# Attention sums scaled by reciprocals that a DMA spreads over the partitions, and turned once instead of twice

## The reference, cut to what matters

```python
scores = scale * (q @ k^T) + bias;  kept: keys of a local window, and a few global keys
scores = scores - max(scores)
a = exp(scores)
a = a / (sum(a, axis=-1) + 1e-9)          # one divisor per query and head
x = (a @ v), heads side by side            # (2, 768, 512)
h = (x^T @ U @ V)^T;  u = x + h            # mixes tokens, rank 32
y = u + relu(u @ w_ch1) @ w_ch2            # 512 -> 2048 -> 512
out = gated unit of y with w_in, w_spatial, b_spatial, w_out
```

## Time and profile before

| what | us |
|---|---|
| median of three runs | 494.83 |
| span of the profiled execution | 493.2 |
| profiled execution beside the median: what lies around the span | 1.6 |
| DVE takes the first sums (step 1), start | 13.84 |
| ACT copies turned exponentials of quad 2 (step 1), start | 15.56 |
| ACT copies turned exponentials of quad 22 (step 22), start | 88.37 |
| first matmul after attention, start | 92.15 |

### The profile page before, as it was taken

One profiled execution on the slowest core, in us unless ns is written; L12 is line 12 of the kernel. 1 busy time (PEld: TensorE's weight loads), 2 busy tenths in 40 slices (PEclk: granted clock), 3 DMA queues, 4 the chain that ended last, 5 costly groups with the idle time before them and its releaser, 6 DMA issues.

```text
span 493.2 us, 7961 instructions
## 1 busy us (share of the span) xinstructions
PE 489.0 (99%) x2804; PEld 409.3 (83%) x2804; DVE 310.2 (63%) x727; ACT 222.0 (45%) x520; POOL 250.2 (51%) x221
## 2 busy tenths in 40 slices
PE   9999999999999999999999999999999999999997
PEld 8788677887888888888888888888888888998986
DVE  5888788421279456564655656557868888878600
ACT  7988889532234633242332322415433356333122
POOL 5997576443346666854566546232885201950000
PEclk9999999999999999999999999999999999999999
DMA  8734501132222322012222020220213000001022
GB/s 236 236 127 111 191 2 45 46 128 86 81 87 89 129 85 71 31 72 85 85 86 78 8 85 3 84 64 2 64 65 115 4 0 1 1 1 43 23 85 108
DMA packets 14697, 36.29 MB, mean 74 GB/s; under 512 B 2496, under 2 KB 2752, under 8 KB 14656
## 3 DMA queue, kind: packets, MB, share of 16 engines
q1 hardware_dynamic: 12640, 32.35, 19.8%
q10 hardware_dynamic: 2016, 3.41, 1.8%
HBM read 32.61 MB, written 3.15 MB: 72 GB/s over the span
## 4 chain that ended last, share of the span: by engine, by line
PE 82%; DVE 6%; POOL 4%; ACT 3%; issue 2%; DVEq 2%; DMA 1%; SPq 0%; ACTq 0%
PE bank L1792 15%; PE bank L1724 9%; PE bank L1644 9%; PE bank L1874 8%; PE bank L1821 8%; PE bank L1814 8%; PE bank L1513 7%; PE bank L1551 4%; PE bank L1569 4%; PE bank L1536 4%; PE bank L1503 1%; POOL sp_op L587 1%; PE bank L1583 1%; DVE newton L1020 1%; DVEq L1008 1%
## 5 line engine op out<-in xcount | busy, mean ns | idle before, releaser
L532 POOL TENSOR_TENSOR w_slot<-stage,w_slot 128x1024 fp32r<-128x1024 f32 x30 | 73.0, 2445 | 65.4 <-ACT w_slot L1249 65.4
L940 DVE TENSOR_TENSOR uT<-bank,uT 128x512 f32<-128x512 f32 x68 | 45.8, 689 | 25.2 <-PE bank L1821 23.2
L1179 ACT ACTIVATE prob<-prob,row_min 128x256 f32<-128x256 f32 (+1 forms) x96 | 45.9, 480 | 6.9 <-DVE row_min L756 6.8
L1792 PE MATMUL bank<-u_op,s_slot 128*128 128x512 f32 x192 | 47.6, 389 | 0.0
L1724 PE MATMUL bank<-hid,w_slot 128*128 128x512 f32 x192 | 46.9, 393 | 0.0
L1644 PE MATMUL bank<-u_split,w_slot 128*128 128x512 f32 x192 | 46.5, 391 | 0.0
L1814 PE MATMUL bank<-hid,w_slot 128*128 128x512 f32 x192 | 46.1, 389 | 0.0
L1821 PE MATMUL bank<-hid,w_slot 128*128 128x512 f32 x192 | 46.1, 389 | 0.0
L978 DVE TENSOR_TENSOR part<-part,bank 128x512 f32<-128x512 f32 x40 | 27.4, 686 | 26.9 <-PE bank L1792 26.5
L1724 PEld LDWEIGHTS bank<-hid,w_slot 128*128 128x128 f32 x192 | 35.7, 188 | 8.2 <-issue 0.9
L1814 PEld LDWEIGHTS bank<-hid,w_slot 128*128 128x128 f32 x192 | 36.0, 188 | 7.5
(11 more groups left out here) (152 smaller groups left out, 963.5 us busy)
## 6 DMA issues: line engine op xcount, KB each, us to landing
stage<-in_w_ch SPq DMA_DIRECT2D x32, 512.0 KB, 3.3
qk_raw<-in_qk SPq DMA_DIRECT2D x23, 256.0 KB, 4.7
v_all<-in_v SPq DMA_DIRECT2D x12, 256.0 KB, 5.2
out_dram<-o_stage ACTq DMA_DIRECT2D x11, 256.0 KB, 2.0
stage<-in_w_spT SPq DMA_DIRECT2D x6, 384.0 KB, 3.1
stage<-in_w_in SPq DMA_DIRECT2D x4, 512.0 KB, 4.2
stage<-in_w_out SPq DMA_DIRECT2D x2, 512.0 KB, 4.0
V_raw<-in_V SPq DMA_DIRECT2D x4, 96.0 KB, 4.6
```

The costliest lines, as they stand in the source:

```text
L532: nc.gpsimd.tensor_tensor(dst[:, LO, :], stage[n % 2][:, 0:w], dst[:, HI, :].bitcast(F32), ALU.subtract).then_inc(w_lo, 1)
L940: vec.tensor_tensor(y, y_bank(e)[:], y, ALU.add).then_inc(y_sum, 1)
L1179: last = sc.activation(prob[r][:, e, 0:w], prob[r][:, e, 0:w], ACT.Exp, bias=row_min[:, k:k + 1], scale=-1.0, accum_out=row_sum[:, q:q + 1])
L1792: last = mm(seven_bank[held][:], lhs, u_op[op][:, m, k, :], start=not more and k == 0 and p == 0, stop=k == 1 and p == 2, skip_group_check ...
```

## The change

The reciprocals of a quad are now made one step earlier, written by a DMA to a scratch tensor in DRAM, and read back by two DMAs that repeat them over 64 partitions each (`inv_rows`, 128 x 256, three buffers). DVE multiplies the bank of sums by them and writes `uT`, dims by tokens, straight away (`scale_x`). PE turns `uT` once to tokens by dims, into the same bank, and ACT copies that to `x_all` (`take_x`). The bank alternates between `o_bank` and `aux`. The first turn and the copy `oT` are gone. The mixing of the first batch moves by one step and to other banks.

```diff
+            def store_inverse(g):
+                sp.wait_ge(inv_ok, g + 1)
+                sp.dma_start(inv_dram[g, :, :].rearrange("k q -> q k"), row_inv[:, g % 4 * 4:g % 4 * 4 + 4],
+                             allow_slow_non_contiguous=True).then_inc(inv_out[g % 2], 16)
+            def spread_inverse(g):
+                sp.wait_ge(inv_out[g % 2], 16 * (g // 2 + 1))
+                if g >= 3:
+                    sp.wait_ge(xT_sb, g - 2)
+                for e in range(2):
+                    rows = slice(e * D, (e + 1) * D)
+                    sp.dma_start(inv_rows[g % 3][rows, :, :],
+                                 inv_dram[g, 2 * e:2 * e + 2, :].partition_broadcast(D)
+                                 ).then_inc(inv_in[g % 3], 16)
...
-                for t in range(3, TILES):
-                    load_qk(t)
-                    load_v(t - 1)
-                    if t == 6:
+                load_qk(3)
+                load_v(2)
+                load_v(3)
+                for g in range(QUADS):
+                    if g == 11:
+                        load_v(NT)
+                    store_inverse(g)
+                    spread_inverse(g)
+                    if g % 2 == 0 and g // 2 + 4 < TILES:
+                        load_qk(g // 2 + 4)
+                    if g in (1, 3):
+                        load_v((g + 7) // 2)
+                    if g % 2 and g >= 11 and (g + 3) // 2 < TILES:
+                        load_v((g + 3) // 2)
+                    if g == 6:
                         load_stage(0)
                         load_stage(1)
...
-            def take_oT(g):
...
-            def take_x(g):
...
+            def scale_x(g):
+                dve.wait_ge(inv_in[g % 3], 32 * (g // 3 + 1))
                 dve.wait_ge(pv_done, g + 1)
+                vec.tensor_tensor(x_tile(g), x_bank(g)[:, 0:256].rearrange("p (c q) -> p c q", c=2),
+                                  inv_rows[g % 3][:], ALU.mult).then_inc(xT_sb, 1)
...
-                    if s >= 1 and s - 1 not in OT_AMID:
-                        take_oT(s - 1)
                     if 0 <= s < QUADS and s != 2:
                         take_probT(s)
                     if s >= 1:
-                        take_x(s - 1)
-                    if 0 <= s < QUADS:
-                        invert(s)
+                        scale_x(s - 1)
+                    if 0 <= s + 1 < QUADS:
+                        invert(s + 1)
...
-            def take_xT(g, after=0):
+            def take_x(g):
                 t, hq = divmod(g, 2)
-                act.wait_ge(xT_ps, g + 1)
-                if after:
-                    act.wait_ge(x_half, after)
+                act.wait_ge(x_ps, g + 1)
+                if t == XS and hq == 0:
+                    act.wait_ge(z_acc, 1)
+                sc.activation(x_all[:, t % XS, hq * 256:hq * 256 + 256], x_bank(g)[:, 0:256],
+                              ACT.Copy).then_inc(x_half, 1)
...
                     if s == 13:
                         split_stage(0)
+                    if s == GATHER:
                         copy_z(0)
+                    if s >= 2:
+                        take_x(s - 2)
                     if 0 <= s + 1 < QUADS:
                         add_eps(s + 1)
...
-                    if s >= 2:
-                        take_xT(s - 2, s)
...
-                    if s in (16, 18, 20, 22):
-                        round_u((s - 16) // 2)
+                    for j in range(FIRST):
+                        if s == MIX_AT[j] + 1:
+                            round_u(j)
...
             def weigh(g):
-                if g:
-                    pe.wait_ge(oT_sb, g)
+                if g >= 2:
+                    pe.wait_ge(x_half, g - 1)
...
-            def turn_o(g):
...
+            def turn_x(g):
+                t, hq = divmod(g, 2)
+                pe.wait_ge(xT_sb, g + 1)
+                for c in range(2):
+                    last = nc.tensor.transpose(x_bank(g)[:, c * P:(c + 1) * P],
+                                               uT[:, 2 * hq + c, t * P:(t + 1) * P], ident[:])
+                last.then_inc(x_ps, 1)
...
```

More of the change, by code:

```diff
@@ L23, with build @@
 MASK_FILL = 1.0e9
-def build(nc, qk, qT, kT, v, cfg, U, V, w_ch, w_in, w_spT, b_sp, w_out, x_dram, out):
+def build(nc, qk, qT, kT, v, cfg, U, V, w_ch, w_in, w_spT, b_sp, w_out, x_dram, inv_dram, out):
     B, DM, S = qT.shape
@@ L161, in build @@
         z_part = at("z_part", [P, DM], F32, SLOT * 11)
-        oT = [at(f"oT{r}", [P, 2, P], F32, SLOT * 11 + 2048 + 1024 * r) for r in range(2)]
+        inv_rows = [at(f"inv_rows{r}", [P, 2, P], F32, SLOT * 11 + 2048 + 1024 * r) for r in range(3)]
         pos_w = SLOT * 11 + 2048
@@ L237, in build, with x_bank, x_tile @@
         FIRST = KD
-        z_bank, fold_bank = (s_bank[0], aux), (s_bank[2], aux)
+        z_bank, fold_bank = (s_bank[2], aux), (s_bank[0], aux)
+        def x_bank(g):
+            return (o_bank, aux)[g % 2]
+        def x_tile(g):
+            t, hq = divmod(g, 2)
+            return uT[:, 2 * hq:2 * hq + 2, t * P:(t + 1) * P]
+        GATHER = 14
+        MIX_AT = (16, 18, 20, 20)
         def mix_bank(j):
             if j < FIRST:
-                return s_bank[0]
+                return s_bank[3 if j == FIRST - 1 else 2]
             return o_bank if j >= 2 * KD and j % 2 else aux
-        OT_AMID = (0, 1, 12)
         def globs_before(g):
@@ L672, in _ @@
                         split_early(1, g // 22)
-                    if g >= 17 and g % 2:
-                        split_u((g - 17) // 2)
+                    for j in range(FIRST):
+                        if g == MIX_AT[j] + 2:
+                            split_u(j)
             with pool.Else():
@@ L885, in _ @@
                         score_bias(s + 2)
-                    if s == 14:
+                    if s == 15:
                         split_z(0)
-                    if s in (15, 17, 19):
-                        sum_u((s - 15) // 2)
-                    if s == 22:
-                        sum_u(FIRST - 1)
+                    for j in range(FIRST):
+                        if s == MIX_AT[j]:
+                            sum_u(j)
             with dve.Else():
@@ L1299, in _ @@
                     round_u(j)
-                for g in range(2 * NT, QUADS - 2):
-                    take_xT(g)
+                for g in range(2 * NT, QUADS):
+                    wide_take_xT(g)
+                act.wait_ge(w_xT, QUADS)
+                act.sem_inc(xT_sb, QUADS)
+                act.sem_inc(x_half, QUADS - 2)
             for f in range(FT):
@@ L1686, in _ @@
                 hidden(0)
-                turn_o(QUADS - 1)
-                pe.wait_ge(x_half, QUADS - 1)
                 turn_x(QUADS - 2)
@@ L1697, in _ @@
                 for g in range(2 * NT):
-                    if g:
-                        pe.wait_ge(xT_sb, g)
-                    turn_x(g)
+                    wide_turn_x(g)
                 pe.wait_ge(U_in, 16)
@@ L1711, in _ @@
                 pe.wait_ge(w_back, 16 * TILES)
-                for g in range(2 * NT, QUADS - 1):
-                    pe.wait_ge(xT_sb, g)
-                    turn_x(g)
+                for g in range(2 * NT, QUADS):
+                    wide_turn_x(g)
                 pe.sem_inc(scored, QUADS)
@@ L1717, in _ @@
                 hidden(0)
+                turn_x(QUADS - 2)
             def contract(f):
```

114 lines of the change are left out of this document (49 added, 65 removed).

## The result

The changed kernel takes 688.15 us (686.03 to 693.37, 4 runs) where the kernel before takes 494.8: a ratio of 1.392, interval 1.387 to 1.397. The forecast was 522 with a range of 505 to 546, so the sign was right and the size was wrong by a factor of seven: +193 us, not +28.

A forecast was written before the change was run, and what follows sets the result against it. PE bounds the kernel before, ACT close below; after the change SP's queue binds quads 1 to 15 (69.5 us), then ACT and DVE. Attention ends at 120.1 against 92.15, +27.9 on 494.8: forecast 522, range 505 to 546.

The forecast's parts named there:

- new order of DVE and ACT: Attention steps: DVE's reciprocals wait for ACT ahead of the next bias; plain step 3.95 us, +13.4 us in all.
- three DMAs in SP's queue: Quads 1 to 15: SP waits for each store, then issues spreads and loads; 4.63 us a quad, +14.5 us.
- the store's landing, 2.6 us: Store of a quad's reciprocals, 512 elements of 4 bytes: 2.6 us to landing, between 1.7 and 5.2.
- upper bound of 5.2: Most a store of reciprocals would take to land, from U's load of 768 pieces of 128 bytes: 5.2 us.
- The other estimate: Store of reciprocals at 2.0 us plus bytes, whatever its pieces: quads 4.03 us, +17.7, 512.5 us in all.
- Rival 1: Attention: ACT and DVE alone are the bound, DMAs hide in the two steps; +13.4, 508 us; chance 0.27.
- Rival 2: Store of reciprocals is as dear as U's load, 5.2 us: 564 us, half way 543; chance 0.11.
- Rival 3: Attention: PE stays the bound and the kernel gets faster, 494.8 - 5.8 = 489 us; chance 0.05.
- Rival 4: Attention: PE's clock falls to 1.2 GHz as it stands still, steps up to 6.3 us: 552 us; chance 0.07.

The follow-up runs named there:

- no DMAs: Changed kernel without the store and spreads of reciprocals; the multiplication takes ones, so the division is left out: 510.88 us, ratio 1.033.
- the filled kernel: Changed kernel with 45 extra matmuls into a free bank in each of 12 steps, where PE waits anyway: 707.35 us.

## Why the prediction was wrong, step by step

The 193.3 us come apart in three parts, by measured times (537.9 is a single run):

| from | to | us | step of the prediction |
|---|---|---|---|
| before, 494.8 | no DMAs, 510.9 | +16.1 | new order of DVE and ACT: +13.4 |
| 510.9 | 512 elements, each in 64 bytes of its own, 537.9 | +27.0 | three DMAs in SP's queue: +14.5 |
| 537.9 | changed kernel, 688.15 | +150.2 | not in it |

**The step that failed** is the term "the store's landing, 2.6 us", with its upper bound of 5.2. It measured 9.3. Its working took a price for each piece from U's load, 1.0 us for 512 pieces, and put 1.7 below it. For pieces that lie 64 bytes apart this came near the measured 3.1 us, in part by luck, as it was the price of a load. What no row of before held was a store whose single elements lie side by side in device memory. I had the layout before me (512 elements, a quad's 128 queries beside each other in device memory, each from another partition) and only counted its pieces. The upper bound came from a load of pieces of 128 bytes; "these are writes of single elements" was worth 0.2 us to me. The bound above wasn't one, and the range rested on it. Two slips in the sums are small beside this: 1.2 us for 768 pieces are 0.8 for 512 and not 1.0, and the steps from 2 to 22 add up to 83.0, not 83.1. The other estimate, a landing of 2.0 and 512.5 in all, was too low as well: no variant of the store had a median under 3.0.

The Trainium skill, DMA: Bandwidth & Descriptors, says in its Specifications that transfers below 512 bytes are done as read-modify-write. The runs add that small writes alone are not dear (512 of them, 64 bytes apart, 3.1 us), and that the same number took 9.3 where they lay side by side; whether read-modify-write is the cause no run shows. Its Rules for kernel authors, cited in the prediction, count a strided last dimension as one descriptor per element: so it was (560 packets under 512 B in the window of the store), but the same count cost 3.1 or 9.3.

**The size of the term.** By the means of the changed kernel a quad is 9.4 from the store's issue to that of the spreads, 1.3 for these (median 1.09, a few are longer) and 0.6 for the loads, so 11.3, against 11.4 measured, the rest being gaps between issues; the prediction's 2.6 + 0.8 + loads and what a store queues behind them made 4.63. And with every quad beyond what ACT and DVE need, all 24 pay it, not 16.

**What was right.** The mechanism: SP's queue waits for its own store, issues two spreads and then the loads, and is the bound; DVE waits in the multiplication, with the bias behind it, and ACT and PE behind that. Moving the loads beside the store's flight (13.0 us) shows it by experiment. The rest of the sum, roughly: with a landing of 3.1 in place of 2.6 (16 x 0.5 = 8), issues of 1.09 for the spreads in place of 0.8 (16 x 0.29 = 4.6) and 1.06 and 0.58 for the loads in place of 0.90 and 0.43 (some 2), 522 becomes 537, and the run with elements apart took 537.9. The parts fit less well than the total: in that run the stores of quads 1 and 16 go out at 18.98 and 100.24 us, 81.3 apart where the prediction had 69.5 (+11.8), and from there to the first matmul behind attention, at 135.43, are 35.2 where it had 32.4, because the queue stayed the bound to the last quad. The issues were dearer than those of loads before.

**Rival 1**, ACT and DVE alone: 508 forecast, 510.9 without the DMAs, with a step of 3.88 against 3.95. It is a true part, and hidden under the queue. **Rival 2**, a store as dear as U's load, 564: the right direction; its 5.2 was too small. **Rival 3**, PE as the bound: its step of 3.17 was shown, but its 489 asked for the saving in every step; with the waits taken away it is 492.5. Besides the handover that the prediction named, it needs the sums kept out of the bank that ACT copies from: the prediction missed that wait. **Rival 4**: the clock did fall, to 0.50 over most of 20 to 290 us, but it priced that with PE as the bound (+30 on 522). PE was not: the filled kernel ran at 1.00 and gained nothing. At the end of the stage the lower clock shows in a row (12 matmuls of line 1679 in 4.85 us, at the high clock 3.06), yet from the last multiplication on the kernel takes only 398.11 - 397.45 = 0.66 us more than before.

```profile
271.51 4.85 PE L1679 MATMUL bank<-u_split,w_slot 128*128 128x512 f32 x12
...
292.24 3.06 PE L1679 MATMUL bank<-u_split,w_slot 128*128 128x512 f32 x12
```

## What to carry to other kernels

Before you price a store by its pieces or bytes, look at how close together its separate writes fall in device memory: 512 single elements of 4 bytes landed in 3.1 us when they lay 64 bytes apart, in 3.8 at 16 bytes and in 9.3 side by side, and the same 2 KB in pieces of 16 bytes in 3.0. If a queue waits for its own DMA and other issues stand behind that wait, put them between the issue and the wait. An upper bound from the nearest row bounds nothing if that row is of another kind, here a load for a store; the range should then be as wide as the ignorance.

## What the runs showed of the hardware that I had not expected

- The time of writes that lie side by side isn't seen as DMA traffic. The packets were through 2.8 us after the issue, and the last 6.3 us before the store counted as landed held a single packet, of another queue (share 0.03, 1 GB/s). Half the elements at the same density took as long (9.1 against 9.3).
- The spreads that read what such a store had written landed in 3.7 us, and in 2.6 where the same 2 KB had come in 16-byte pieces. Whether it is the reads that are slower or the other traffic beside them wasn't tried.
- With PE busy 127 of 250 us in the changed kernel's stage the granted clock was 0.56 on average there; with filler, busy 138.6 of 140, it was 1.00. The window of the changed kernel:

```profile
20.00:270.00 250.00, 127.25 (x790) 96.20 (x792) 54.38 (x239) 65.77 (x240) 55.33 (x75) 0.56 0.22 42
```
